# The last three token tiles walk through the weight chunks together, and the slot sums are divided behind the output weights

## The reference

```python
gate = 1.0 / (1.0 + np.exp(-(x @ w_gate)))          # x: 2304 x 512, w_gate, w_val: 512 x 1536
x = (gate * (x @ w_val)) @ w_out                    # 2304 x 512
logits = x @ phi                                    # 2304 x 32
d = np.exp(logits - logits.max(0))                  # softmax over the tokens, for each slot
slot_input = (d / (d.sum(0) + 1e-09)).T @ x         # 32 x 512
for e in range(8):                                  # 4 slots an expert, w1: 512 x 1024, w2: 1024 x 512
    slot_out[e] = np.maximum(slot_input[e] @ w1[e], 0.0) @ w2[e]
c = np.exp(logits - logits.max(1))                  # softmax over the slots, for each token
out = (c / (c.sum(1) + 1e-09)) @ slot_out
```

## Time and profile before

| | us |
|---|---|
| median of 3 runs | 609.86 |
| the runs | 606.81, 609.86, 611.08 |
| the profiled execution | 607.04 |
| its span, first to last instruction | 605.3 |
| TensorE busy | 554.4 (92%) |
| VectorE, ScalarE, GpSimd busy | 225.5, 200.8, 100.2 |
| DMA | 70.97 MB, mean 117 GB/s |

### The profile page before, as it was taken

How to read it: one execution, slowest core, us unless ns; L and a number is a source line. 1 busy time by engine, 2 the same in 40 slices (tenths; PEclk the granted TensorE clock), 3 DMA queues, 4 the chain that set the end, 5 groups by cost and what they waited for, 6 DMA issues and landing times.

```text
span 605.3 us, 11206 instructions
## 1 busy us (share of the span) xinstructions
PE 554.4 (92%) x4455; PEld 415.6 (69%) x4455; DVE 225.5 (37%) x504; ACT 200.8 (33%) x511; POOL 100.2 (17%) x171
## 2 busy tenths in 40 slices
PE   5687999999999999999999999999999999869963
PEld 4575777776777778777877877787777877624421
DVE  3495843425624252444234335432213112120213
ACT  4354654343343323252324333332222221211113
POOL 7554021132230202121111203010000000000000
PEclk9797799999999999999999999999999999978988
DMA  8879541212311111111020300003300307999958
GB/s 205 209 203 224 164 107 45 59 40 48 77 52 29 43 40 40 42 41 42 24 58 1 70 12 28 16 22 131 148 1 1 139 1 259 396 363 396 398 204 312
DMA packets 86708, 70.97 MB, mean 117 GB/s; under 512 B 61313, under 2 KB 65921, under 8 KB 86657
## 3 DMA queue, kind: packets, MB, share of 16 engines
q1 hardware_dynamic: 86656, 70.25, 37.5%
HBM read 65.52 MB, written 4.72 MB: 116 GB/s over the span
## 4 chain that ended last, share of the span: by engine, by line
PE 84%; DMA 6%; DVE 4%; ACT 2%; issue 2%; SPq 1%; DVEq 0%
PE gateb L897 26%; PE valb L897 25%; PE unitb L905 4%; PE unitb L854 3%; DMA ew_low<-in_moe_w_dram 3%; PE unitb L810 3%; PE unitb L926 2%; PE unitb L817 2%; PE unitb L845 2%; PE unitb L912 2%; PE unitb L972 2%; PE unitb L825 2%; DMA qtok<-in_q_dram 2%; PE unitb L832 2%; PE gateb L990 1%
## 5 line engine op out<-in xcount | busy, mean ns | idle before, releaser
L897 PE MATMUL gateb<-w_hl,xhl 128*128 128x512 f32 x648 | 162.8, 400 | 0.0
L897 PE MATMUL valb<-w_hl,xhl 128*128 128x512 f32 x648 | 161.5, 398 | 0.0
L897 PEld LDWEIGHTS gateb<-w_hl,xhl 128*128 128x128 f32 x648 | 119.0, 189 | 32.9 <-issue 8.7
L897 PEld LDWEIGHTS valb<-w_hl,xhl 128*128 128x128 f32 x648 | 117.9, 188 | 23.0
L628 ACT ACTIVATE hid<-gateb 128x512 f32<-128x512 f32 x54 | 32.3, 597 | 177.1 <-PE gateb L897 174.0
L744 DVE SCALAR_TENSOR_TENSOR hid<-hid,valb 128x512 f32<-128x512 f32 x54 | 37.1, 688 | 126.4 <-PE valb L897 126.3
L546 POOL TENSOR_TENSOR vd<-v 72x256 f32<-72x256 f32 x16 | 12.1, 756 | 173.2 <-PE unitb L838 168.3
L557 ACT ACTIVATE hT<-unitb 128x512 f32<-128x512 f32 x54 | 32.1, 594 | 13.2 <-PE unitb L905 12.9
L727 DVE TENSOR_TENSOR xraw<-unitb,outd 128x192 f32<-128x192 f32 x43 | 15.0, 355 | 56.2 <-PE unitb L854 56.0
L905 PE MATMUL unitb<-ident,hid 128*128 128x128 f32 x216 | 33.2, 276 | 1.1 <-DVE hid L744 0.4
L905 PEld LDWEIGHTS unitb<-ident,hid 128*128 128x128 f32 x216 | 25.0, 140 | 6.1 <-issue 2.3
(11 more groups left out here) (180 smaller groups left out, 665.6 us busy)
## 6 DMA issues: line engine op xcount, KB each, us to landing
ew_low<-in_moe_w_dram SPq DMA_DIRECT2D x19, 1024.0 KB, 14.3
ew_high<-in_moe_w_dram SPq DMA_DIRECT2D x13, 1024.0 KB, 13.5
qtok<-in_q_dram SPq DMA_DIRECT2D x32, 144.0 KB, 2.9
ktok<-in_k_dram SPq DMA_DIRECT2D x32, 144.0 KB, 3.2
v<-in_v_dram SPq DMA_DIRECT2D x32, 144.0 KB
out_dram<-outs SPq DMA_DIRECT2D x18, 256.0 KB, 3.0
vloc<-in_v_dram SPq DMA_DIRECT2D x32, 112.0 KB
xraw<-in_moe_w_out_dram SPq DMA_DIRECT2D x12, 256.0 KB, 3.7
```

The lines of the kernel that those rows point to most:

```text
L897: last = mm(bank[:, :], xhl[:, i % NX, x, kk, :], w_hl[:, c, m, w, kk, :], start=j == 0, stop=j == len(order) - 1)
```

## The change

Four things are edited together.

1. The last three tiles (15, 16 and 17) go through chunk 0, then chunk 1, then chunk 2. In chunk 0 each tile has its gate and its val, in the other two the order is gate, val of tile 15, gates of 16 and 17, vals of 16 and 17. The splits of x for these tiles come at tile 14, and there are four buffers for a split x (`NX`) where there were three.
2. The groups of the running softmax are pairs for tiles 0 to 13, then tile 14 alone, tile 15 alone, and tiles 16 and 17. The last LG is cut in two steps with one bank: `LG0` has the first two chunks, `LG` the third. The transpositions of tile 16 are held back until the LG of tile 15 has read `hT`. The running maximum is kept negated, which saves an instruction.
3. The multiplication of `acc` with 1/(2 sum) is gone. VectorE multiplies `sin`, the product with w_out, by it while copying it out of PSUM, which ScalarE did as a plain copy. In the last group VectorE adds to `acc` before it makes the combine weights.
4. `SPARE` columns are put behind `xraw`, so that the expert tiles' places fall on the halves of `w_hl`'s chunks, and `hT` lies ahead of `hid`. `wait_place` follows: tiles on `xhl` wait for the last val, tiles on `hT` for the last LG.

```diff
-    t0, t1 = tiles - 2, tiles - 1
+    t0 = tiles - 3
     ff = [(name, (i, c)) for i in range(t0) for c in range(chunks) for name in ("gate", "val")]
-    ff += [(name, (i, c)) for i in (t0, t1) for c in range(chunks - 1) for name in ("gate", "val")]
-    ff += [(name, (i, chunks - 1)) for name in ("gate", "val") for i in (t0, t1)]
+    ff += [(name, (i, 0)) for i in range(t0, tiles) for name in ("gate", "val")]
+    for c in range(1, chunks):
+        ff += [("gate", (t0, c)), ("val", (t0, c)), ("gate", (t0 + 1, c)), ("gate", (t0 + 2, c)), ("val", (t0 + 1, c)),
+               ("val", (t0 + 2, c))]
...
+                       (5, ("ELT", g + 1), ("LG0", g + 2), ("TR", (t0 + 2, last_c)), ("SL", g + 1)),
...
+    GROUPS = [(i, GT) for i in range(0, TILES - 4, GT)] + [(TILES - 4, 1), (TILES - 3, 1), (TILES - 2, GT)]
...
-    NX = 3
+    NX = 4
...
+        SPARE = -(ATT_BYTES + X_BYTES) % (4 * HALF_TILE)
...
             sp.wait_ge(x_lo, TILES)
-            if end <= ATT_BYTES + X_BYTES:
+            end -= ATT_BYTES + X_BYTES + SPARE
+            if end <= 0:
                 return
             for c in range(FC):
                 for m, ready in enumerate((gate_ready, val_ready)):
-                    if end <= ATT_BYTES + X_BYTES + c * W_BYTES + (m + 1) * W_BYTES // 2:
+                    if end <= c * W_BYTES + (m + 1) * W_BYTES // 2:
                         sp.wait_ge(ready, ff_n[TILES - 1, c] + 1)
                         return
+            end -= FC * W_BYTES
+            sp.wait_ge(val_ready, FC * TILES)
+            if end <= XHL_BYTES:
+                return
+            if end <= XHL_BYTES + HT_BYTES:
+                wait_unit(sp, ("LG", GROUPS_T - 1))
+                return
             wait_banks(sp)
...
         def pe_tail(pe):
             wait_token_phases(pe)
-            pe.wait_ge(acc_norm, 1)
...
-            act.wait_ge(sin_ready, 1)
-            copy(sin[:, :], sin_b[:, :]).then_inc(sin_done, 1)
...
         def dve_tail(dve):
             dve.wait_ge(slot_sum, GROUPS_T)
-            nc.vector.tensor_scalar(slot_inv[:, 0:1], run_sum[:], EPS, None, ALU.add).then_inc(inv_step, 1)
+
+            nc.vector.tensor_scalar(slot_inv[:, 0:1], run_sum[:], EPS, 2.0, ALU.add, ALU.mult).then_inc(inv_step, 1)
             dve.wait_ge(inv_step, 1)
             nc.vector.reciprocal(slot_inv[:, 1:2], slot_inv[:, 0:1]).then_inc(inv_step, 1)
+            wait_token_phases(dve)
+            nc.vector.memset(hTe[:], 0.0).then_inc(hT_zero, 1)
             dve.wait_ge(inv_step, 2)
-            wait_token_phases(dve)
-
-            nc.vector.tensor_scalar(acc[:, :], acc[:, :], slot_inv[:, 1:2], 0.5, ALU.mult, ALU.mult).then_inc(acc_norm, 1)
-            nc.vector.memset(hTe[:], 0.0).then_inc(hT_zero, 1)
+            dve.wait_ge(sin_ready, 1)
+            nc.vector.tensor_scalar(sin[:, :], sin_b[:, :], slot_inv[:, 1:2], None, ALU.mult).then_inc(sin_done, 1)
```

More of the change, by code:

```diff
@@ L54, in attention_steps, with program_steps @@
     return out
-def program_steps(tiles, chunks, batch_tokens, pairs, heads_of, w_pieces, wo_pieces):
+def program_steps(tiles, chunks, groups, batch_tokens, pairs, heads_of, w_pieces, wo_pieces):
     turns = [*zip((-2, -1, 0), FIRST_TURNS)] + [(p, HEAD_TURN) for p in range(1, heads_of - 1)] + \
@@ L115, in program_steps @@
         put(place_of[("gate", (i, 0))] - 2 if i < t0 else place_of[("gate", (t0 - 1, 0))] + i - t0, ("xs", i))
-    for i in range(tiles):
+    for i in range(t0):
         for c in range(chunks):
             put(place_of[("val", (i, c))] + 1, ("TR", (i, c)))
[L119 to L123, removed]
+    for g, (first, size) in enumerate(groups):
+        n = place_of[("val", (first + size - 1, chunks - 1))]
+        if first + size < t0:
+            for at, name in ((2, "LG"), (3, "LS"), (5, "ELT"), (6, "SL")):
+                put(n + at, (name, g))
+    last_c, g = chunks - 1, len(groups) - 3
+    n = place_of[("gate", (t0, 0))]
+    for at, *those in ((1, ("LG", g)), (2, ("LS", g)), (3, ("ELT", g), ("TR", (t0, 0)), ("SL", g)), (5, ("TR", (t0 + 2, 0)))):
+        put(n + at, *those)
+    for c in range(1, last_c):
+        n = place_of[("gate", (t0, c))]
+        put(n + 2, ("TR", (t0, c)))
+        put(n + 5, ("TR", (t0 + 2, c)))
+    n = place_of[("gate", (t0, last_c))]
+    for at, *those in ((2, ("TR", (t0, last_c))), (3, ("LG", g + 1)), (4, ("LS", g + 1), *[("TR", (t0 + 1, c)) for c in range(chunks)]),
+                       (5, ("ELT", g + 1), ("LG0", g + 2), ("TR", (t0 + 2, last_c)), ("SL", g + 1)),
+                       (6, ("LG", g + 2)), (7, ("LS", g + 2)), (8, ("ELT", g + 2)), (9, ("SL", g + 2))):
+        put(n + at, *those)
     body = []
@@ L189, in build @@
     GT = 2
-    GROUPS_T = TILES // GT
+    GROUPS = [(i, GT) for i in range(0, TILES - 4, GT)] + [(TILES - 4, 1), (TILES - 3, 1), (TILES - 2, GT)]
+    GROUPS_T = len(GROUPS)
+    group_of = {first + t: (g, t) for g, (first, size) in enumerate(GROUPS) for t in range(size)}
     RING = 2 * S
-    NX = 3
+    NX = 4
     NH = 3
-    assert HP == KT and NS == 32 and D == QT and CG * NS == P and RING % P == 0 and TILES % GT == 0
+    assert HP == KT and NS == 32 and D == QT and CG * NS == P and RING % P == 0 and len(group_of) == TILES
     def key_start(t):
@@ L206, in build, with hT_before @@
     assert [arg for name, arg in body if name == "val"] == list(ff_n)
-    last_of = {}
-    for n, s in enumerate(steps):
-        last_of[s] = n
+    def hT_before(i):
+        g, t = group_of[i]
+        return max((n for n in range(g) if GROUPS[n][1] > t), default=None)
     ctx = ExitStack()
@@ L262, in build @@
         xraw = sb("xraw", [P, KT, RING], where=tokens)
+        sb("spare", [P, SPARE // 4], where=tokens)
         arriving = ExitStack()
@@ L301, in build @@
         hs = sb("hs", [P, 2, GC], where=tail)
-        hTe = sb("hTe", [P, 2, GC // P, GROUPS, NS], where=tail)
+        hTe = sb("hTe", [P, 2, GC // P, UP_GROUPS, NS], where=tail)
         shT = sb("shT", [P, FK * NS], where=tail)
@@ L767, in dve_step, with add_up @@
                                         ALU.subtract).then_inc(free, 1)
             elif name == "SL":
+                def add_up():
+                    wait_unit(dve, s)
+                    nc.vector.scalar_tensor_tensor(out=acc[:, :], in0=acc[:, :], scalar=alpha[:], in1=ub[:, 0:SW],
+                                                   op0=ALU.mult, op1=ALU.add).then_inc(free, 1)
+                first, size = GROUPS[arg]
+                if arg == GROUPS_T - 1:
+                    add_up()
@@ L970, in up @@
                 for kk in range(KT):
-                    for j in range(GROUPS):
+                    for j in range(UP_GROUPS):
                         last = mm(up_b[e % 2][j * NS:(j + 1) * NS, 0:GC], sT[:, kk, :],
```

126 lines of the change are left out of this document (73 added, 53 removed).

## The result

The changed kernel takes 600.93 us in the median of four runs (599.31 to 604.20) against 609.62 for the kernel before (606.81 to 611.08): a ratio of 0.9885, interval 0.9853 to 0.9916. 599.9 was forecast, with 595.5 to 605.0. Two more series of the same kernel gave 0.9867 (0.9827 to 0.9907) and 0.9844 (0.9809 to 0.9879). It is faster by 1.2 to 1.6%. The recorded ratios are not the quotients of the medians, which would be 0.986 in the first series.

A forecast was written before the change was run, and what follows sets the result against it. The prediction held that the expert phase waits for its last weights, dated by the stream's start. Terms 6.77 + 1.67 + 0.2 = 8.6 us, taken from the 608.45 median, gave 599.9 us, range 595.5 to 605.

The forecast's parts named there:

- The bound: Expert phase: it waits for its last weights, whose date is set by when the stream of loads began.
- The wait of 5.01 and the cold 1.76: Last up-projection: the 5.01 us wait for weights and 1.76 us of cold clock both go, worth 6.77 us.
- What frees the transfers: Expert loads: earlier release (chunk 0 at 483.3, not 501.9) and new places leave 18 tiles at the last val.
- The margin: Last expert tiles: tiles 29 and 31 land 4.9 and 4.2 us before TensorE wants them; TensorE is late next.
- rival D: Tail of the experts: bound by transfers again, 1 to 3 us of the 6.77 remain, 602; 7%.
- The chain: Last val to slot inputs ready: shorter by 0.67 + 0.08 + 1.0 - 0.08 = 1.67 us.
- The token phase: TensorE's work ahead of the last val: -0.2 us, range -0.4 to +1.1, last val ending at 523.8.
- idle of TensorE within 470 to 524: Sign of a wrong prediction, end of the token phase: the order of three tiles would then wait for ScalarE's copies.
- The other sign: Sign of a wrong prediction, end of the expert loads: the last `ew_low` landing after 576.
- A: SyncE's queue: one entry still waiting late holds all behind it, early release fails, 608.4, no change; 5%.
- C: Expert phase stays at half clock: 3.2 us per cold expert, slower from three on, 619 with six; 4%.
- B: Serial chain: the clock takes part of the gain, two more cold stretches of 1.8 each, 603.4; 12%.

The follow-up runs named there:

- places_only: Kernel before with part 4 alone (spare columns, hT ahead of hid, new release rules), order and groups as before; 602.71 us, ratio 0.9868.
- hold_chunk2: Changed kernel with all loads of tiles 4 and later held until the gate of tile 15 on chunk 2; 609.31 us, ratio 0.9995.
- division_only: Kernel before with the division behind w_out alone, VectorE's order in the last group left as it was; 607.35 us, ratio 0.995.
- places_division: Kernel before with part 4 (places) and the division behind w_out; 603.02 us, ratio 0.9903.
- the second pair: Both kernels profiled again, nothing edited: the kernel before at 609.52 us, ratio 1.0006, and the changed kernel at 601.26 us, ratio 0.9867.
- tr_later: Changed kernel with the transposition of tile 17 in chunks 0 and 1 one matmul group later; 597.41 us, ratio 0.9783, and again 598.09 us, ratio 0.9825.
- division_again: Second run of the kernel before with the division behind w_out alone; 608.67 us, ratio 0.9994.
- the third profile: The changed kernel itself, unedited, profiled a third time; 598.38 us, ratio 0.9844.
- order_only: Changed kernel without part 4 (no spare columns, hid ahead of hT, old release rules); 610.39 us, ratio 1.001.

## Why the prediction was right, and where it was not

**The bound: right.** The end of the experts is set by the arrival of the last weights. `places_only` changes nothing but the places and dates of the loads and takes 5.3 off the segment behind the last val, `hold_chunk2` moves nothing but the loads and costs 8.9. `division_only` and `places_division` shorten the chain and gain nothing.

**The wait of 5.01 and the cold 1.76: right in size.** The expert phase went from 42.93 and 42.73 to 36.48 and 36.50: 6.2 to 6.5 against 6.77. In the first pair 5.01 + 1.76 are there in full; 0.52 is lost again because the first up-projection took 3.64 for 3.12, by the clock, and 0.20 gained at the transposition behind it (0.44 for 0.64).

**What frees the transfers: half right.** The text had two causes side by side, the earlier release by the order of three tiles and the places. By themselves they aren't of one kind. From the load of w_out to the end of the experts the places alone take off 5.2 of the 6.3 us (170.82, 165.65, 164.52), and parts 1 to 3 without them none (172.79). The release of chunk 0 at 484 instead of 502, with which the step began, is not worth its 18 us: the pairs land and then the transfers lie idle (54 GB/s at 520, 79 at 528) until the last val, since no more places are free. It isn't worth nothing either, for `hold_chunk2`, where the same eight tiles go 6 to 25 us later, counted from the load of w_out, pays 8.9. What counts is how many tiles are left at the last val and whether they can go without the banks. With the places the rest of the change is then worth something: behind the last val 54.9 against 58.2, and 54.1 with the old division. But 2.2 of these 3.3 it paid in stalls.

**The margin: too large.** I gave 4.9 and 4.2 us of room, with 1.5 us for a stream's start and landing together. The runs show about 4 us for the two (72.2 - 68.4 and 43.9 - 39.5). Tile 29 was to land 43.6 behind the last val; where TensorE waits for it, it is used at 46.7, and tile 31 at 51.9 to 52.0, where 48.8 was said. In the first changed profile TensorE comes for them at 48.4 and 53.0, so the room is 1.7 and 1.1. So the changed kernel is not freed from its transfers but close to balance with them: with a cold chain TensorE ends last, with a warm one it waits 2.46 at the end. "What is late next is TensorE itself" held in two of three profiles, and rival D, the tail bound by transfers again, came up in the third.

**The chain: nearly right in the sum, with the help of the clock.** Forecast 1.67; measured 2.05 and, against the second pair, 2.71. In the first pair the first LG step gave 0.80 (3.91 to 3.11) for 0.67, and the steps from there to SL 0.15 for 0.08. The division gave 0.52 for 0.92: between `acc` and its transposition there is not 0.14 but 0.36 us, and VectorE's product out of PSUM took 0.76, not 0.68. That makes 1.47. The other 0.58 is clock, which falls elsewhere by chance: SL 1.88 for 2.82, against the transposition of `acc` at 0.89 for 0.53.

**The token phase: the step that failed.** I had -0.2 with -0.4 to +1.1 and it is +2.20 to +2.23, in all three profiles. I counted matmuls and not what each waits for. The text said of the waits only that TensorE had no idle there before, and that what `hid` owes the transposition is 0.86 behind the last val; that the same 0.86 applies wherever TR stands right behind its own val, in chunks 0 and 1, was in the order of steps and I did not look for it there. Each costs 0.87 of wait and some 0.2 more, and `tr_later` takes away 2.07. What is left for the extra groups is +0.13 (107.51 against 107.38). The prediction named idle of TensorE within 470 to 524 as a sign of being wrong, and it came; but the wait is for VectorE's multiply and not, as was said there, for ScalarE's copies. The other sign, a last `ew_low` behind 576, came too, by little: about 580, less 3.45.

**The rivals.** A fell: the releases came as written. C fell: between the first and the last expert the changed kernel's up-projections take 1.86 in all three profiles. A cold down-projection, which C priced at up to 1.96 more, took 2.74 for 1.72 in `division_again`. B came in part: the cold stretches of chain and first up-projection vary from none to three, but the warm chain of the third profile gained only 0.2 (54.74 for 54.94), since TensorE then waited for the transfers.

**The sum.** From the load of w_out to the end, 188.7 and 189.1 became 182.3, 182.4 and 182.2: 6.3 to 6.9, where 8.6 were forecast. The missing 2 us are the token phase, 2.4 beside its forecast, and nearly all of that the stalls. The forecast of 599.9 missed the median of 600.93 by 1.0, and that is better than its terms deserve. The medians lie 8.7 apart and the ratio makes it 7.0, where the traces show 6.3 to 6.9 behind the load of w_out, and ahead of it no gain: the two kernels' first profiles differ there by 3.45 the other way. Where the rest of the medians' difference lies no trace shows; that it made up for the 2.3 by which the forecast gain exceeds the first pair's is chance.

The fastest version that was run is `tr_later`, 597.41 and 598.09.

## What to carry to other kernels

When the end waits for a long stream of loads, ask first how many of them can't be started until the last phase ends, and what holds each of them; an earlier release upstream of that point is worth only what it lets through before then, and beyond that it moves an idle gap. Behind a reordering look at every step that now follows directly the one that makes its input: the latency of the engine between them, here 0.87, appears each time. And cut the spans of both profiles at common marks before explaining their difference, for a part that the change doesn't touch can differ by more than the gain.

## What the runs showed of the hardware

A full stream of 1 MB loads costs 2.63 us each (28 in some 74 us in `hold_chunk2`), plus about 4 us once from the first issue to the use of the tile that is waited for (3.8 in `hold_chunk2`, 4.4 in `order_only`). A matmul group that stood right behind the val whose product it needs waited 0.87 us for VectorE's multiply of 128x512 and then took 0.63 for 0.44. And TensorE's clock fell to 1.2 GHz ahead of the loads, at 96 to 108 and 124 to 132, in one execution of the changed kernel (mean granted clock 0.86 and 0.79; 0.50 in the windows 101 to 104 and 129 to 131) and not in another (1.00), with the load of w_out 3.35 us apart. In the 4 us ahead of the first fall, 96 to 100, TensorE was busy for 2.51 us in both.
